# Fused attention and expert layers on one core: the last 64 keys of two heads share one transpose

## What is computed

```python
B, H, S, D = 2, 8, 576, 64
scores = q @ k.T / sqrt(D)
kth    = the 32nd largest score of each row
attn   = softmax(where(scores >= kth, scores, -1e9))
x = attn @ v                          # to 1152 x 512
x = (x @ w_a) * (x @ w_b) @ w_out     # 512 -> 1536 -> 512
for e in range(4):                    # 512 -> 1024 -> 512
    out += p[:, e:e+1] * (relu(x @ w1[e]) @ w2[e])
```

## Time and profile before

| | us |
|---|---|
| runs | 848.16, 848.91, 845.84 (median 848.16) |
| profiled execution | 849.11 |
| its span, first to last instruction | 847.3 |
| around the span | 1.8 |
| PE matmul busy | 807.8 (95%) |
| DVE busy | 457.9 (54%) |
| ACT busy | 384.6 (45%) |
| POOL busy | 297.1 (35%) |
| mean granted TensorE clock | 0.972 of full |

### The profile page before, as it was taken

How to read it: one execution, slowest core, us unless ns; L and a number is a source line. 1 busy time by engine, 2 the same in 40 slices (tenths; PEclk the granted TensorE clock), 3 DMA queues, 4 the chain that set the end, 5 groups by cost and what they waited for, 6 DMA issues and landing times.

```text
span 847.3 us, 13113 instructions
## 1 busy us (share of the span) xinstructions
PE 807.8 (95%) x4985; PEld 713.1 (84%) x4985; DVE 457.9 (54%) x902; ACT 384.6 (45%) x712; POOL 297.1 (35%) x269
## 2 busy tenths in 40 slices
PE   4468999999999999999999999999999999999998
PEld 3346788888888888888889899899899898898996
DVE  5979999899999999998124112122121121221121
ACT  5665787777777777777444011311032010230110
POOL 3766875454545454545331000530016000440000
PEclk9557999999999999999999999999999999999999
DMA  9540685456545654445688500230004100000000
GB/s 233 160 117 1 219 242 206 150 193 200 187 148 183 254 170 158 163 155 173 209 285 300 219 1 1 99 100 1 1 1 141 58 1 1 1 1 38 14 25 38
DMA packets 71631, 102.59 MB, mean 121 GB/s; under 512 B 32528, under 2 KB 48912, under 8 KB 71568
## 3 DMA queue, kind: packets, MB, share of 16 engines
q1 hardware_dynamic: 70512, 101.48, 36.6%
q10 hardware_dynamic: 1056, 0.26, 0.2%
HBM read 88.36 MB, written 13.37 MB: 120 GB/s over the span
## 4 chain that ended last, share of the span: by engine, by line
PE 88%; ACT 4%; POOL 4%; issue 2%; DMA 1%; DVE 1%; SPq 0%; ACTq 0%; POOLq 0%
PE ps L612 24%; PE ps L632 23%; PE ps L522 16%; PE ps L507 8%; PE ps L471 5%; PE ps L442 5%; PE ps L451 4%; PE ps L480 1%; POOL p_sb L1007 1%; ACT p_sb L702 1%; POOL wa_lo L1041 1%; DMA wo<-wo_d 1%; PE ps L402 1%; ACT pT L709 1%; PE ps L514 0%
## 5 line engine op out<-in xcount | busy, mean ns | idle before, releaser
L769 ACT ACTIVATE h_hi<-ps 128x384 fp32r<-128x384 f32 x96 | 47.0, 491 | 269.7 <-PE ps L612 269.5
L874 DVE MAX8 m<-work 128x8 f32<-128x576 f32 x216 | 152.3, 747 | 0.0
L1057 POOL TENSOR_TENSOR w_lo<-w_raw,w_hi 128x2048 fp32r<-128x2048 f32 x12 | 55.1, 4617 | 244.5 <-ACT w_hi L765 244.5
L933 DVE SCALAR_TENSOR_TENSOR h_lo<-ps,h_hi 128x384 fp32r<-128x384 f32 x96 | 53.3, 557 | 156.8 <-ACT h_hi L769 156.8
L612 PE MATMUL ps<-x_hi,w_hi 128*128 128x384 f32 x384 | 129.0, 336 | 0.0
L612 PE MATMUL ps<-x_hi,w_lo 128*128 128x384 f32 x384 | 128.8, 336 | 0.0
L612 PE MATMUL ps<-x_lo,w_hi 128*128 128x384 f32 x384 | 128.8, 335 | 0.0
L632 PE MATMUL ps<-w_hi,h_hi 128*128 128x512 f32 x288 | 112.2, 390 | 0.0
L632 PE MATMUL ps<-w_hi,h_lo 128*128 128x512 f32 x288 | 112.2, 390 | 0.0
L632 PE MATMUL ps<-w_lo,h_hi 128*128 128x512 f32 x288 | 112.1, 389 | 0.0
L880 DVE MATCH_REPLACE8 work<-m,work 128x576 f32<-128x576 f32 x144 | 106.0, 743 | 0.0
(11 more groups left out here) (90 smaller groups left out, 1507.8 us busy)
## 6 DMA issues: line engine op xcount, KB each, us to landing
wo<-wo_d SPq DMA_DIRECT2D x96, 512.0 KB, 4.9
w_raw<-moe_w_in SPq DMA_DIRECT2D x16, 1024.0 KB, 6.6
wo_d<-wo SPq DMA_DIRECT2D x12, 512.0 KB, 4.5
w_raw<-moe_w_a_in SPq DMA_DIRECT2D x4, 768.0 KB, 6.0
w_raw<-moe_w_b_in SPq DMA_DIRECT2D x4, 768.0 KB, 5.5
wo_raw<-moe_w_out_in SPq DMA_DIRECT2D x12, 256.0 KB, 3.9
v_sb<-v_in SPq DMA_DIRECT2D x18, 128.0 KB, 3.8
x_d<-x_hi_out SPq DMA_DIRECT2D x9, 256.0 KB, 3.0
```

The lines of the kernel that those rows point to most:

```text
L769: copy(h_hi[:, m, :], ps[:, UP + m % FREE_UP, 0:GN], ACT.Relu).then_inc(ac_r, 1)
L874: nc.vector.max(m8[:, par, i, 8 * r:8 * r + 8], work[:, i, :]).then_inc(ve_top, 1)
L933: nc.vector.scalar_tensor_tensor(h_lo[:, m, :], ps[:, UP + m % FREE_UP, 0:GN], 0.0, h_hi[:, m, :].bitcast(F32), ALU.max, ALU.subtract).the ...
L1057: nc.gpsimd.tensor_tensor(lo[:, s, :], raw[s][:], hi[:, s, :].bitcast(F32), ALU.subtract).then_inc(done, 1)
```

## The change

p of a pair is stored as one row of 1152 columns without gaps: the even head's 576 keys in order, then the odd head's keys turned round by 64 columns, its last 64 keys first. The last 64 keys of both heads are then neighbours in columns 512 to 639, and one transpose brings the even head's to partitions 0 to 63 and the odd head's to 64 to 127. There are nine transposes per unit. The odd head's half of `kT` is stored turned round in the same way, which takes two copies of 64 partitions where one of 128 did it. The odd heads' last v rows go to partitions 64 to 127. The fifth chunk of the weighted sum uses 64 rows of PE per head. The zeros are no longer needed.

```diff
-        p_sb = sb("p_sb", [P, 2, KC * P])
+        p_sb = sb("p_sb", [P, 2, S])
+        p_row = p_sb[:].rearrange("p h s -> p (h s)")
...
-                src = v[b, :, (KC - 1) * P:S, :].rearrange("h s d -> s h d")
-                sp.dma_start(v_sb[b][0:KL, KC - 1, :, :], src).then_inc(ld_v[b], 16)
+                for side in range(2):
+                    src = v[b, :, (KC - 1) * P:S, :].rearrange("(r z) s d -> z s r d", z=2)[side]
+                    dst = v_sb[b][side * KL:(side + 1) * KL, KC - 1, :, :].rearrange("p (r z) d -> p z r d", z=2)[:, side]
+                    sp.dma_start(dst, src).then_inc(ld_v[b], 16)
...
             def scores(n):
                 if n == 0:
                     pe.wait_ge(ac_q, 1)
+                    pe.wait_ge(ve_k, 2)
...
             def p_transpose(n):
-                    for c in range(KC):
+                    first = head * (S + KL)
+                    for c in range(KC - 1):
                         tr = nc.tensor.transpose(ps_pT[head][:, c * P:(c + 1) * P],
-                                                 p_sb[:, head, c * P:(c + 1) * P], ident[:])
+                                                 p_row[:, first + c * P:first + (c + 1) * P], ident[:])
+                    if head:
+                        tr = nc.tensor.transpose(ps_pT[1][:, (KC - 1) * P:KC * P], p_row[:, S - KL:S + KL], ident[:])
                     tr.then_inc(pe_pT, 1)
...
             def weighted_sum(n):
-                    pe.wait_ge(ve_z, 2)
...
+                            rows = slice(0, P) if c < KC - 1 else slice(head * KL, (head + 1) * KL)
                             mm = nc.tensor.matmul(ps_x[head * D:(head + 1) * D, pr * P + tok.start:pr * P + tok.stop],
-                                                  v_sb[b][:, c, 2 * pr + head, :], pT[:, head, c, tok],
+                                                  v_sb[b][rows, c, 2 * pr + head, :], pT[rows, head if c < KC - 1 else 1, c, tok],
                                                   start=c == 0, stop=c == KC - 1)
...
-            pe.wait_ge(po_id, 3)
+            pe.wait_ge(po_id, 2)
...
             def keys_pair(b, pr):
-                copy(kT[:, b, pr, 0:(KC - 1) * P], bank, ACT.Copy).then_inc(ac_k, 1)
+                even = copy(kT[0:D, b, pr, 0:S - KL], bank[0:D, :], ACT.Copy)
+                if (b, pr) == (0, 0):
+                    even.then_inc(ac_k, 1)
+                else:
+                    copy(kT[D:P, b, pr, KL:S], bank[D:P, :], ACT.Copy).then_inc(ac_k, 1)
...
             def keys_tail(b, first, last, count):
-                copy(kT[:, b, first:last, (KC - 1) * P:S], bank.rearrange("p (r s) -> p r s", s=KL), ACT.Copy).then_inc(ac_k, 1)
+                turned = bank.rearrange("p (r s) -> p r s", s=KL)
+                even = copy(kT[0:D, b, first:last, S - KL:S], turned[0:D], ACT.Copy)
+                if (b, first) == (0, 0):
+                    even.then_inc(ac_k, 1)
+                else:
+                    copy(kT[D:P, b, first:last, 0:KL], turned[D:P], ACT.Copy).then_inc(ac_k, 1)
...
             def p_out(n):
+                    chunks = KC - 1 + head
-                    copy(pT[:, head, :, :], ps_pT[head][:, 0:KC * P].rearrange("p (c t) -> p c t", c=KC),
+                    copy(pT[:, head, 0:chunks, :], ps_pT[head][:, 0:chunks * P].rearrange("p (c t) -> p c t", c=chunks),
                          ACT.Copy).then_inc(ac_pT, 1)
...
+            dve.wait_ge(pe_k, 1)
+            nc.vector.tensor_copy(kT[D:P, 0, 0, KL:S], ps_a[D:P, :]).then_inc(ve_k, 1)
+            dve.wait_ge(pe_k, 2)
+            nc.vector.tensor_copy(kT[D:P, 0, 0, 0:KL], ps_y[D:P, 0:KL]).then_inc(ve_k, 1)
...
-            nc.vector.memset(v_sb[0][KL:P, KC - 1, :, :], 0.0)
-            nc.vector.memset(v_sb[1][KL:P, KC - 1, :, :], 0.0).then_inc(ve_z, 1)
...
-            nc.gpsimd.memset(p_sb[:, :, S:KC * P], 0.0).then_inc(po_id, 1)
```

More of the change, by code:

```diff
@@ L182, in build @@
         ac_w1, ac_w2, ac_r = sem("ac_w1"), sem("ac_w2"), sem("ac_r")
-        ve_z, ve_top, ve_den, ve_xu, ve_xT, ve_pr = (sem(n) for n in ("ve_z", "ve_top", "ve_den", "ve_xu", "ve_xT", "ve_pr"))
+        ve_z, ve_k, ve_top, ve_den, ve_xu, ve_xT, ve_pr = (sem(n) for n in ("ve_z", "ve_k", "ve_top", "ve_den", "ve_xu", "ve_xT", "ve_pr"))
         ve_w1, ve_w2, ve_hl, ve_acc = (sem(n) for n in ("ve_w1", "ve_w2", "ve_hl", "ve_acc"))
@@ L457, in weighted_sum @@
                 if n == 0:
-                    pe.wait_ge(ld_v[0], 16 * (H + 1))
-                    pe.wait_ge(ve_z, 2)
+                    pe.wait_ge(ld_v[0], 16 * (H + 2))
                 if n == SPLIT * PR:
-                    pe.wait_ge(ld_v[1], 16 * (H + 1))
+                    pe.wait_ge(ld_v[1], 16 * (H + 2))
                 if pr == 0:
@@ L691, in below_top @@
                     act.wait_ge(pe_pT, 2 * n - 1 + head)
-                copy(p_sb[:, head, 0:S], s_sb[:, (2 * n + head) % 4, :], ACT.Relu, scale=-STEEP,
+                copy(p_sb[:, head, :], s_sb[:, (2 * n + head) % 4, :], ACT.Relu, scale=-STEEP,
                      bias=kbig[:, n % 2, head:head + 1]).then_inc(ac_u, 1)
@@ L696, in exponentials @@
                 t, h = n // PR, 2 * (n % PR) + head
-                slot = p_sb[:, head, 0:S]
+                slot = p_sb[:, head, :]
                 act.wait_ge(po_p, 2 * n + head + 1)
@@ L1006, in push_down @@
                 pool.wait_ge(ac_u, 2 * n + head + 1)
-                nc.gpsimd.tensor_tensor(p_sb[:, head, 0:S], s_sb[:, (2 * n + head) % 4, :], p_sb[:, head, 0:S],
+                nc.gpsimd.tensor_tensor(p_sb[:, head, :], s_sb[:, (2 * n + head) % 4, :], p_sb[:, head, :],
                                         ALU.subtract).then_inc(po_p, 1)
```

## The result

| | before | changed |
|---|---|---|
| median of 7 runs, us | 846.26 | 850.38 |
| lowest to highest | 844.95 to 848.91 | 849.08 to 851.92 |
| profiled execution, us | 849.11 | 849.08 |
| ratio, 95% interval | | 1.0046 (1.0028 to 1.0064) |

The change makes the kernel slower by 3.9 us, between 2.4 and 5.4. The forecast was 3.2 more (0.4%), and the range holds the measured time.

A forecast was written before the change was run, and what follows sets the result against it. PE was taken to bound units 8 to 35, the chain of waits before. -3.05 + 5.4 + 0.55 + 0.1 (first slots) + 0.2 = 3.2 us more: 852.3 profiled, 851.4 against the median; range 845.5 to 857.

The forecast's parts named there:

- The bound: Attention slots from about 101 us to 416 us: PE sets the pace at 10.70 us a slot, DVE second.
- Transposes: One of ten transposes a unit goes, 0.109 us each, in 28 PE-bound units: 3.05 us less.
- Shapes: Weighted sum's fifth chunk adds one change of array shape a unit, 0.15 us, three in tile 4: 5.4 us more.
- half-clock slots: First slots: a change of shape costs 0.27 us in each of three weighted sums on the chain: 0.8 us more.
- Rival A: PE narrows the array's rows without emptying, so changes of shape cost nothing: 3.0 us less, 845.2; chance 0.22.
- Rival B: In the fifth chunk the two heads take turns instead of running side by side: 10.6 us more, 858.8; chance 0.15.
- Rival C: Clock granted some 3 us earlier or later, around 63 to 80 us: 1 to 3 us either side; chance 0.08.
- The keys of batch 1: Slots 10, 11, 13, 14: ACT's second half copy hidden by a hair; 0.2 us more, between nothing and 1.2.
- The start: ACT copies k pairs 1 to 3 in halves; PE waits for pair 1's second half: 0.55 us more.
- The first slots' gain: At half clock, shorter copies of pT save 0.5 us and one transpose fewer 0.2 us.
- The sum: All terms of the forecast together: 3.2 us more, 0.4%.

The follow-up runs named there:

- number 5: Changed kernel with the odd head's short chunk its first 64 keys (keys copied whole, in order) and the fifth chunk on 128 rows with zeros in v_sb; 0.9946 of before.
- number 1: Kernel before with only the fifth chunk of the weighted sum on 64 rows of PE, rows 0 to 63 for both heads, ten transposes; 1.0040 of before.
- number 6: Changed kernel with its 64*64 chunk third of five in the weighted sum instead of last; 1.0095 of before.
- number 7: Changed kernel with its 64*64 chunk first of five in the weighted sum instead of last; 1.0040 of before.
- the changed kernel's second profile: Profile of a second build of the changed kernel, measured again with nothing altered; 1.0041 of before.
- number 3: Kernel before with only the key copies split into two halves of 64 partitions, into the old places; 1.0014 of before.
- number 4: Changed kernel without the turning: the odd head's short chunk is its first 64 keys, keys copied whole, fifth chunk still 64*64; 0.9997 of before.
- number 10: Changed kernel with only batch 1's keys turned round; batch 0's stay in order and are copied whole at the start; 1.0018 of before.
- number 2: Changed kernel with the fifth chunk back on all 128 rows and zeros in v_sb; nine transposes, keys still turned; 0.9972 of before.
- number 8: Changed kernel with unit 1's scores ahead of pair 3's key transposes on PE, ACT's copies in the same order; 1.0042 of before.
- number 9: The kernel of number 5 with unit 1's scores ahead of pair 3's key transposes, ACT's copies in the same order; 0.9955 of before.

## Why the prediction was right, and where it was not

**The bound** was read rightly in the main: PE nearly without a gap from about 101 us on, DVE second with room. Time taken from PE came back in full (number 5: 2.99 for 2.83), and time added to it cost nearly in full (number 1: 3.94 of 4.38, because PE lost 0.1 us in five slots before). The longest wait of a PE matmul in the changed kernel between 101 and 416 us is 1.0 us, once.

**Transposes:** 0.109 each, 3.05 for 28 units; measured 2.99 for 26.

**Shapes:** the step that decided the sign. One transition in tile 4's scores had priced it at 0.15, and the chain in the changed kernel, number 1 and number 6 gave 0.15 each. The sum was 5.4 for 28 units, which is 22 x 0.15 + 4 x 0.45 = 5.1 for the 26 of the stretch; measured 3.94 (number 1). The direction came out right, the size over a quarter too large. What the prediction passed over is that the scores of tile 4 are 64*64 themselves: "64*64 goes over to 64*128, in place of 128*64 to 64*128, one for one" fails four times, 0.64 us. Of the 0.5 that is left, 0.1 is tile 4's sum (0.43 for 0.45 each); the other 0.4 is in the five slots in which PE was not as full as "busy without a gap" says. In the half-clock slots I expected 0.8 more, three sums at 0.27 each. The traces show 0.20 a sum, and in number 1 and the changed kernel the second of the three ran at full clock. The rest shows no such loss between before and number 1 (571.6 and 571.4), to the 1 us or so that runs allow.

**Rival A** (going over costs nothing) falls by number 1. **Rival B** (the two heads take turns) falls by the trace: 1.39, not 1.6. The Trainium skill, "TensorEngine Tiling (Array Packing)", Key Properties, says a change of tiling mode drains TensorE; numbers 1, 6 and 7 agree, at 0.15 us a time and nothing where the mode stays. The same page of the Trainium skill warns under PSUM Pressure that different row tiles cannot access one bank at the same time. Here the two heads do write one bank from different rows, in different halves of the partitions, and their time is that of work side by side: 1.39 us, as in number 1, where both heads use the same rows.

**Rival C** (the clock) shows in the profiles and is not settled for the run. The send of slot 9 begins at 115.87 us in before, at 114.27 in the changed kernel and at 116.74 in the changed kernel's second profile. So two executions of one kernel differ there by 2.5 us, more than before and the changed kernel do (1.6). No run separates an effect of the change on the clock from this spread, and the missing sum of the single parts above may lie here.

**The keys of batch 1** were put at 0.2, and cost 1.0 in number 3 (0.57 in the stretch, 0.41 in slot 10) and 0.6 in the change against number 4. Within the stated bound, but the reading was wrong: half copies follow each other by 0.60 us, not by 0.50, so "hidden by a hair" fails, and slot 10 with its four half copies was named only in the bound.

**The start** is the mis-sized term: 0.55 forecast for it, some 2 to 3 measured (number 10 against the two measurements of the changed kernel). I followed PE from pair 1's second half to unit 1's scores, and that came true to 0.2 us (13.47 for 13.3). I left out two things. ACT's own halves for pairs 2 and 3 end at 14.77, ahead of those scores' copy and the weight slices. And the scores took 1.05 us longer than before, so that ACT waited 1.04 for them. The first weight slice began 1.8 later. In numbers 2, 7 and 8, which have the halves but scores of 1.24 us, it begins at 15.70 to 16.16, and with whole copies at 14.27 to 15.11: about 1.3 us come with the halves alone. The first slots' gain fits what was forecast, within the 1 us that the rest is good to: the rest with nine transposes is 0.3 to 1.4 below that with ten, at whole copies (numbers 4, 5, 9 and 10 against 571.4 and 571.6); 0.7 was expected (0.5 for the copies and 0.2 for the transposes).

**The sum** came out near (3.2 and 3.9) partly by luck. The stretch was forecast about 2.5 longer (2.83 less, 5.1 and 0.2 more) and is 1.64 longer; what lies outside it was forecast some 0.7 longer and is about 2.3. The two misses, 0.8 too much and 1.6 too little, nearly cancel.

## What to carry to other kernels

Count changes of PE's tile shape in the order of its matmuls like instructions: here each is 0.15 us, more than the 0.109 us transpose that was saved, and a chunk kept whole with zeros was cheaper than one cut to its rows. When two halves must meet, first ask which of the orders the data may have: the first 64 keys did as well as the last, and nothing had to be turned. An engine with much room on average can be on the chain at the start: key copies doubled there cost some 2 to 3 us, though ACT is busy 45% of the span.

## What was not expected of the hardware

Two matmuls on 64*64 parts of the array, one after another from different stages, show no gap, while 128*64 to 64*64 shows 0.15 us each time, though the columns stay. And the granted clock moved between executions of nearly the same kernel: the weighted sum of unit 1 ran at half clock in before's profile (2.40 us, at 41.74) and at full in the changed kernel's (1.46, at 43.50); the granted clock is 0.50 and 1.00 there. The granted clock does not tell everything either: in the second profile of the changed kernel it reads 1.00 from 16 to 36 us, and the sum at 33.55 takes 2.60 us, as where it reads 0.50. In the traces taken, unit 1's scores, the first after PE's short idle at 12 us, took 1.24 us where they began at up to 13.33 us and 2.29 where they began at 13.47 or later. One trace alone of such a start is not enough to compare by.
